# Another split of the last token tile, and later loads of the first expert's weights, in a fused attention, experts and SoLU kernel

## What is computed

```
# 1. attention, 2 batches x 8 heads, 768 positions, head size 64;
#    8 global keys and a causal window of 96, bias by distance
scores = scale * q @ k.T + bias;  a = softmax(where(keep, scores, -1e9));  x = a @ v

# 2. four experts, all of them on every token: 1536 tokens, 512 -> 1024 -> 512
p = domain_probs / (sum(domain_probs) + 1e-9)
out = sum over e of p[:, e] * (relu(x @ w1[e]) @ w2[e])

# 3. SoLU with layer norm
h = out @ w_in;  s = h * softmax(h);  ln = (s - mean(s)) / sqrt(var(s) + 1e-6) * g_ln
result = ln @ w_out                      # 1536 x 512
```

## Time and profile before

| what | us |
|---|---|
| median of 3 runs (745.72 to 745.82) | 745.74 |
| the profiled execution, as timed | 746.49 |
| its span in the profile | 744.6 |
| TensorE busy | 739.6 (99%) |
| VectorE busy | 515.3 (69%) |
| GpSimd busy | 348.3 (47%) |
| ScalarE busy | 224.5 (30%) |
| TensorE's granted clock, all 40 slices of the span | 0.9 or more of full speed |

### The profile page before, as it was taken

How to read it: one execution, slowest core, us unless ns; L and a number is a source line. 1 busy time by engine, 2 the same in 40 slices (tenths; PEclk the granted TensorE clock), 3 DMA queues, 4 the chain that set the end, 5 groups by cost and what they waited for, 6 DMA issues and landing times.

```text
span 744.6 us, 12548 instructions
## 1 busy us (share of the span) xinstructions
PE 739.6 (99%) x3992; PEld 650.6 (87%) x3992; DVE 515.3 (69%) x1031; ACT 224.5 (30%) x422; POOL 348.3 (47%) x334
## 2 busy tenths in 40 slices
PE   9999999999999999999999999999999999999998
PEld 7888899889898988888998989989898888888887
DVE  5777777676666766767666676666668858767773
ACT  6667741111111111111111111111115465433332
POOL 3558446153542535435263352644519986442400
PEclk9999999999999999999999999999999999999999
DMA  9735300110101000010000101000030200000001
GB/s 257 206 108 148 106 30 1 57 29 29 35 21 56 28 28 28 28 56 28 28 28 28 56 18 38 28 28 0 1 114 9 106 0 15 15 29 28 15 30 42
DMA packets 38226, 36.11 MB, mean 48 GB/s; under 512 B 14512, under 2 KB 31152, under 8 KB 38192
## 3 DMA queue, kind: packets, MB, share of 16 engines
q1 hardware_dynamic: 36448, 33.46, 14.7%
q10 hardware_dynamic: 1744, 2.23, 0.9%
HBM read 32.54 MB, written 3.15 MB: 48 GB/s over the span
## 4 chain that ended last, share of the span: by engine, by line
PE 95%; DVE 2%; DMA 1%; SPq 1%; issue 1%; ACT 0%; POOL 0%; DVEq 0%
PE y_ps L879 35%; PE p_ps L859 31%; PE o_ps L926 5%; PE up_ps L1097 3%; PE up_ps L1096 3%; PE up_ps L1098 3%; PE s_ps L897 3%; PE pT_ps L907 3%; PE out_ps L1126 2%; PE out_ps L1128 2%; PE out_ps L1127 2%; DMA qk<-in_qkW 1%; PE lnT_ps L1111 1%; PE xt_ps L937 1%; PE xr_ps L1020 1%
## 5 line engine op out<-in xcount | busy, mean ns | idle before, releaser
L879 PE MATMUL y_ps<-w2s,hs 128*128 128x512 f32 x1140 | 286.0, 395 | 0.3 <-DVE acc L1591 0.3
L859 PE MATMUL p_ps<-xs,ws 128*128 128x384 f32 x1344 | 255.2, 336 | 0.0
L879 PEld LDWEIGHTS y_ps<-w2s,hs 128*128 128x128 f32 x1140 | 212.2, 188 | 41.3 <-DVE acc L1591 0.9
L859 PEld LDWEIGHTS p_ps<-xs,ws 128*128 128x128 f32 x1344 | 237.5, 188 | 11.0
L1591 DVE SCALAR_TENSOR_TENSOR acc<-y_ps,pr,acc 128x512 f32<-128x512 f32 x178 | 132.9, 748 | 79.8 <-PE y_ps L879 79.1
L1205 ACT ACTIVATE hs<-hs_sum 128x384 fp32r<-128x384 f32 x128 | 67.3, 526 | 353.0 <-DVE hs_sum L1556 233.7
L1575 DVE SCALAR_TENSOR_TENSOR hs<-hs_sum,hs 128x384 fp32r<-128x384 f32 x128 | 97.2, 769 | 4.3 <-ACT hs L1205 2.3
L640 POOL TENSOR_TENSOR ws_sum<-raw_sum 128x256 f32<-128x256 f32 x16 | 11.8, 738 | 146.0 <-PE p_ps L859 146.0
L671 POOL CAST w2s<-raw_sum 128x1024 fp32r<-128x1024 f32 x16 | 16.9, 1055 | 86.3 <-PE y_ps L879 86.3
L1218 ACT ACTIVATE neg_s<-neg_s,row 128x256 f32<-128x256 f32 (+1 forms) x96 | 42.0, 482 | 24.8 <-DVE row L1611 24.5
L1611 DVE CUSTOM_DVE_ANT_0 neg_s<-s_ps,bias 128x256 f32<-128x256 f32 (+1 forms) x87 | 31.2, 398 | 17.7 <-PE s_ps L897 16.4
(11 more groups left out here) (200 smaller groups left out, 977.0 us busy)
## 6 DMA issues: line engine op xcount, KB each, us to landing
raw_sum<-in_w SPq DMA_DIRECT2D x28, 512.0 KB, 3.5
qk<-in_qkW SPq DMA_DIRECT2D x16, 256.0 KB, 3.5
qk<-in_qkW SPq DMA_DIRECT2D x31, 128.0 KB, 3.6
v_sb<-in_v SPq DMA_DIRECT2D x16, 192.0 KB, 3.4
out<-o_sb SPq DMA_DIRECT2D x11, 256.0 KB, 2.0
raw_sum<-in_w ACTq DMA_DIRECT2D x4, 512.0 KB, 9.3
raw_sum<-in_w_in SPq DMA_DIRECT2D x1, 2048.0 KB, 7.8
wout_lo_a_sum<-in_w_out SPq DMA_DIRECT2D x1, 1792.0 KB, 7.6
```

The lines of the kernel that those rows point to most:

```text
L859: mm = nc.tensor.matmul(bank, ws[slot][:, w, part, kk, :], xs[:, 2 * bt + kk, x, part, :], start=(kk == 0 and w == 1 and x == 1), stop=(kk ...
L879: mm = nc.tensor.matmul(mixed_at(s, t), hs[ring][:, h, b, tok], w2s[slot][:, w, f, :], start=(f == 0 and h == 1 and w == 1), stop=(f == 1 ...
```

## The change

1. `last_down`, `last_out`, ScalarE's last two copies and SP's last two stores take the last token tile's 512 output columns as 384 and 128 (`SPLIT = 3 * P`, new function `last_columns`) and no longer as 256 and 256.
2. The four loads of the first expert's weights are two functions now. In the attention of short windows, w1 of group 0 is issued after step b = 3, and w2 of group 0 and both of group 1 after step b = 5, at the end of the first iteration. (`attend_wide`, another path, is not taken with these inputs.)

```diff
+    SPLIT = 3 * P
...
         def last_out(part):
-            return xr_ps[:, 0:DM // 2] if part else out_ps[1][:, 0:DM // 2]
+            return xr_ps[:, 0:DM - SPLIT] if part else out_ps[1][:, 0:SPLIT]
+
+        def last_columns(part):
+            return slice(SPLIT, DM) if part else slice(0, SPLIT)
...
             for part in range(2):
-                cols = slice(part * DM // 2, (part + 1) * DM // 2)
+                cols = last_columns(part)
                 sp.wait_ge(out_copied, TT + part)
                 sp.dma_start(out[(TT - 1) * P:, cols], o_sb[:, 1, cols]).then_inc(out_stored[1], 16)
...
-                cols = slice(part * DM // 2, (part + 1) * DM // 2)
+                cols = last_columns(part)
                 for c in range(FC):
                     nc.tensor.matmul(last_out(part), ln_hi[1][:, c, :], wout_hi(c)[:, cols], start=(c == 0), stop=False)
...
             def attend():
                 for b in range(BL):
-                    if b in (2, 4):
-                        load_first_weights((2, 4).index(b))
                     attention_step(0, b)
+                    if b == 3:
+                        load_first_w1(0)
+                load_first_w2(0)
+                load_first_w1(1)
+                load_first_w2(1)
                 with act.Fori(1, OUTER) as j:
...
-                nc.scalar.activation(o_sb[:, 1, part * DM // 2:(part + 1) * DM // 2], last_out(part), ACT.Copy
+                nc.scalar.activation(o_sb[:, 1, last_columns(part)], last_out(part), ACT.Copy
```

More of the change, by code:

```diff
@@ L1186, in _, with load_first_w1 @@
         def _(act):
-            def load_first_weights(g):
+            def load_first_w1(g):
                 act.dma_start(raw[:, g, :].rearrange("p (k f) -> p k f", k=KC),
@@ L1191, in load_first_weights, with load_first_w2 @@
                               ).then_inc(w1_loaded[g], 16)
+            def load_first_w2(g):
                 act.dma_start(raw[:, 2 + g, :].rearrange("p (f n) -> p f n", f=2),
@@ L1296, in attend_wide @@
                 for g in range(2):
-                    load_first_weights(g)
+                    load_first_w1(g)
+                    load_first_w2(g)
                 with act.Fori(0, R) as r:
```

## The result

| | us |
|---|---|
| before, median of 22 runs (745.71 to 746.86) | 745.93 |
| after, median of 22 runs (746.57 to 747.80) | 746.79 |
| ratio, 95% interval | 1.0012, 1.0006 to 1.0017 |
| profiled execution before, after | 746.49, 746.59 |
| its span before, after | 744.6, 744.7 |

The change costs 0.86 us by the medians. That is inside the 0.2% I had called no change, yet its interval leaves out 1. The two profiled executions differ by 0.10 us only, and this gap between a pair of profiles and two sets of runs is what the study is about. Ratios compare executions at the full granted clock; one of e7, 759.43 us at a clock of 0.984, is left out.

The account below looks back on a forecast made before the run. TensorE, busy for 99% of the span, was taken to bound the kernel. The column split at +0.84 us and the later loads at -0.75 summed to +0.09, giving 745.8 us from a 745.74 median, range 744.5 to 749.0.

Parts of the forecast that it names:

- likeliest case: Last tile's 128-column matmuls run at the weight-load pace, 0.108 us each: 745.8 us, own range 745.6 to 746.9, chance 48%.
- First part: Last token tile, first 24 matmuls: 384 columns in place of 256 cost 0.1733 against 0.1188 us each, +1.31 us.
- Second part: Last token tile, last 24 matmuls: 128 columns in place of 256 take 0.108 against 0.119 us each, -0.26 us.
- Copy and store: After the last matmul: the smaller last copy saves 0.11 us and the smaller last store 0.10 us.
- The stall: Start of the kernel: later weight loads remove TensorE's 0.88 us wait for qk[5]; gain 0.62 to 0.88, taken as -0.75 us.
- The late loads: ScalarE's queue, first iteration: the three late issues fit into 0.8 us of room before TensorE's transpose, costing nothing.
- Columns alone count: Rival on the last tile: a 128-column matmul takes 0.064 us, sum -0.96 us, 744.8 us; chance 18%.
- Priced like f32: Rival on the last tile: 128-column fp32r matmuls cost at least 0.216 us each, sum +2.7 us, 748.4 us; chance 30%.
- The late loads cost more than the early ones: Rival at the start: later loads bring nothing or cost up to 0.5 us, 746.6 to 747.1; 4% together with anything else.

Follow-up runs that it names:

- e7: The kernel before with all four loads of the first expert's weights issued ahead of step b = 1: 747.54 us, ratio 1.0022.
- e9: The kernel before with the last tile as 384 and 128, the second part using 64 of its 128 stationary columns: 745.89 us, ratio 0.9999.
- e2: The kernel before with only the later weight loads, last tile as 256 and 256: 746.05 us, ratio 1.0001.
- e11: The kernel before with only the later weight loads, last tile 256 and 256, measured a second time: 745.89 us, ratio 1.0002.
- e8: The whole change run and profiled once more, against the kernel before: 746.88 us, ratio 1.0012.
- e1: The kernel before with only the last tile split into 384 and 128 columns, weights loaded as before: 746.89 us, ratio 1.0011.
- e3: The kernel before, unchanged, profiled once more: 745.87 us, ratio 0.9999.
- e10: The kernel before with the later loads and 8 warm-up matmuls in place of 10, last tile 256 and 256: 745.83 us, ratio 0.9999.

## Why the prediction was right and where it was off

The time lies in the range (744.5 to 749.0) and in the likeliest case's own (745.6 to 746.9), and the case forecast is the one that happened. The sum was off: +0.09 forecast, +0.86 measured. The likeliest case held it only because its upper end took in no gain at all at the start, and a whole range of 4.5 us would have held many other accounts too; that "no change" came out is owed to an error of 0.77 us being small beside the 1.5 us that it allows.

- **First part, +1.31.** Measured 4.21 us for 24 matmuls, 739.15 - 736.30 = 2.85 before: +1.36. Right.
- **Second part, -0.26.** Measured 2.66 in place of 2.87: -0.21. Right, with its cause: the value products with 65 columns and 0.108 us foretold 0.111, though they are f32 and these are fp32r. e9 shows that it is the weight load. The Trainium skill ("TensorE: Matmul & The Clock Gate", section "LDWEIGHTS (loading the stationary operand)") prices a load at its columns divided by 1.2 ns; by that estimate 128 columns take 107 ns, close to the measured 111, and 64 take 53, where e9 shows 61 (which its moving columns may set).
- **Copy and store, -0.21.** Measured -0.11 and about -0.1. Right.
- **The stall, -0.75.** The step that failed. In the pair of profiles the stall went, and the second iteration began at 23.03 us (forecast 23.0 to 23.2), the profiled time +0.10 against +0.09. There the term was even too small: 0.96 us with the later start taken out, above my 0.62 to 0.88. The 0.26 us that I feared to lose again were not lost: from the scores of qk[5] to the next iteration it is 23.03 - 18.99 = 4.04 us, as in the stalled execution. But I wrote that "the same terms apply" to the median, and this one does not: of eight profiles with the old loads one has the stall, and e2 and e11, the later loads alone, measure +0.10 and -0.03 us. The sign that I passed over was in the table of times: the profiled execution lay 0.75 us above a median whose three runs agree within 0.1 us, about the size of the stall. Had the stall been in those runs too, that distance would have had to come from somewhere else. It is a sign and no proof: the profile of e8 lies 0.46 us above its own median and has no stall. Without this term the forecast is +0.84 us, with the measured sizes of the others +1.36 - 0.21 - 0.11 - 0.10 = +0.94; the runs gave +0.86, and +0.98 in e8 and +0.94 in e1.
- **The late loads, 0.** Right: 0.62 of 0.8 us of room were left.
- **Rivals.** *Columns alone count*: out, 0.111 and not 0.064. *Priced like f32*: out; 24 records of 0.111 us for 24 matmuls. I gave it 30% with no row that spoke for it but the lack of a counterexample. *The late loads cost more than the early ones*: the 746.79 us lie in its 746.6 to 747.1 as well as in the likeliest case, and edit 2 does bring nothing. But its reason, ScalarE's room used up, did not come about: 0.62 us of it were left, and the whole change is no slower than the split with the old loads (ratios 1.0012 and 1.0011).

## What to carry to other kernels

Once a matmul streams fewer moving columns than cover the load of its weights, taking more away saves nothing: move columns between two matmul groups only while both stay above that point, here between 192 and 256 moving columns for fp32r with 128 weight columns. A wait that appears once in one profile, on a DMA, is worth its length only if the timed runs contain it: hold the profiled time against the median before counting on it, and profile the same kernel twice. Executions that start unequally are compared from a point behind the start. Moving transfers out of a crowded stretch pays only where something waited for them in the usual run.

## What was not expected

The start differs between executions of one kernel by up to 0.7 us. The warm-up's 20 records took 3.89 us in the profile of before and 4.61 in e8, and the scores of step b = 2 began at 8.26 and 8.95 us. For before and then for e8, four records of the same scores, and a window (us, TensorE busy and its records, PEclk, DMA share, GB/s):

```profile
4.92 0.60 PE L897 MATMUL o_ps<-qk 64*128 64x256 f32 x4
...
4.00:5.00 1.00, 1.00 (x12) 1.00 1.04 358
```

```profile
5.90 1.03 PE L902 MATMUL o_ps<-qk 64*128 64x256 f32 x4
...
4.00:5.00 1.00, 1.00 (x7) 1.00 1.03 323
```

The pace has risen before 4.92 us in the one and not yet at 5.90 us in the other, while the column of the granted clock reads 1.00 in both. The Trainium skill says of TensorE that it starts at the lower of its two rates and that the moment of the rise differs from run to run ("TensorE: Matmul & The Clock Gate", Part 1); the rise fits, though these rows do not show the clock. That it is the clock is therefore not shown.

By the scores of step b = 3 the start is over. Those of before, of after and of e8:

```profile
11.64 0.93 PE L897 MATMUL s_ps<-qk 64*128 64x128 f32 x8
```

```profile
11.78 0.93 PE L902 MATMUL s_ps<-qk 64*128 64x128 f32 x8
```

```profile
12.57 0.93 PE L902 MATMUL s_ps<-qk 64*128 64x128 f32 x8
```

If their start is subtracted from each profiled time, the executions line up: 733.96 (e3), 733.94 (e2), 733.88 (e11) and 733.88 us (e10) for 256 and 256 columns, 734.81 (after), 734.82 (e1) and 734.77 (e8) for 384 and 128. The profile of before, with its stall, has 734.85; less the 0.96 us that it lost at the stall it has 733.89. The split costs 0.81 to 0.94 us by this count, where the medians gave 0.86 to 0.98, and the later loads nothing. e8 came to these scores 0.79 us after the first profile of the same kernel, and took 0.75 us longer.
